# Weights times V in an attention kernel: one 128-column product, or two 64-column products into two halves of the PSUM partitions

## The reference, cut to what matters

```python
def _attn_ref(q, k, v, proj):            # q, k, v: (2, 8, 768, 64) float32
    q_bits = (np.einsum('bhsd,dk->bhsk', q, proj) > 0)
    k_bits = (np.einsum('bhsd,dk->bhsk', k, proj) > 0)
    ...                                  # six bits make a bucket number
    mask = q_bucket[:, :, :, None] == k_bucket[:, :, None, :]
    scores = scale * np.matmul(q, k.transpose(0, 1, 3, 2))
    scores = np.where(mask, scores, -1000000000.0)
    scores = scores - np.max(scores, axis=-1, keepdims=True)
    attn = np.exp(scores)
    attn = attn / (np.sum(attn, axis=-1, keepdims=True) + 1e-09)
    return np.matmul(attn, v)            # the product that is changed

def reference(...):
    attn_out = _attn_ref(...)            # 16 heads of 768 x 64
    x = attn_out.transpose(0, 2, 1, 3).reshape(B * S, H * D)    # 1536 tokens x 512
    x = _moe_ref(x=x, ...)               # 512 -> 1024, SoLU, layer norm, -> 512
    return _moe2_ref(x=x, ...)           # eight experts, 512 -> 1024 -> 512
```

## Time and profile before

| | us |
|---|---|
| device time, median of 3 runs | 761.47 |
| the three runs | 761.47, 760.52, 2372.37 |
| profiled execution, from its first to its last instruction | 759.0 |
| TensorE busy in it | 662.9 (87%) |
| VectorE busy in it | 496.5 (65%) |
| ScalarE / GpSimd busy | 345.8 / 273.6 |
| `values` (L456): 384 matmul instructions | 134.0 busy |
| `attended` (L720): 32 copies | 540 to 561 ns each |

### The profile page before, as it was taken

The page is one execution under the profiler, slowest core; times in us unless marked ns, Lnnn a source line. Parts: engine busy times, 40 slices in busy tenths (PEclk is TensorE's granted clock), DMA queues, the critical chain, the costliest instruction groups (busy, mean ns, idle before and its releaser), DMA issues.

```text
span 759.0 us, 11820 instructions
## 1 busy us (share of the span) xinstructions
PE 662.9 (87%) x3190; PEld 515.1 (68%) x3191; DVE 496.5 (65%) x931; ACT 345.8 (46%) x563; POOL 273.6 (36%) x185
## 2 busy tenths in 40 slices
PE   3899999999999998899999999850499999999994
PEld 1666666666666666677888888630378878788783
DVE  5788888888888888746565656645234556465621
ACT  2566666666666665552222222322234545454520
POOL 2566666655555554523132222456100010101011
PEclk9899999999999999999999999965599999999998
DMA  9933333333332232003000000035544475656400
GB/s 262 280 99 98 98 97 97 97 97 97 96 97 88 87 87 63 1 1 111 1 1 0 0 0 0 0 116 215 196 167 133 158 251 167 222 174 247 145 17 27
DMA packets 35419, 79.48 MB, mean 105 GB/s; under 512 B 6461, under 2 KB 6589, under 8 KB 35392
## 3 DMA queue, kind: packets, MB, share of 16 engines
q1 hardware_dynamic: 28112, 67.97, 28.7%
q10 hardware_dynamic: 5040, 4.87, 2.4%
q0 software_dynamic: 2240, 6.31, 2.2%
HBM read 67.82 MB, written 12.35 MB: 106 GB/s over the span
## 4 chain that ended last, share of the span: by engine, by line
PE 58%; DVE 21%; issue 10%; POOL 3%; ACT 3%; DMA 2%; ACTq 1%; DVEq 1%; SPq 0%; POOLq 0%
PE PS L439 7%; PE PS L418 7%; DVE sb_nm L681 6%; PE PS L612 4%; PE PS L614 3%; PE PS L613 3%; PE PS L593 3%; PE PS L594 3%; PE PS L595 3%; PE PS L524 3%; PE PS L471 3%; PE PS L473 3%; PE PS L472 3%; PE PS L526 3%; PE PS L525 3%
## 5 line engine op out<-in xcount | busy, mean ns | idle before, releaser
L1200 POOL TENSOR_TENSOR at_P<-at_P,sb_rr 128x768 f32<-128x768 f32 x80 | 121.8, 1530 | 115.6 <-DVE sb_rr L693 115.6
L456 PE MATMUL PS<-at_PT,at_V 128*128 128x384 f32 x384 | 134.0, 486 | 0.0
L991 ACT ACTIVATE at_P<-PS,sb_nb,sb_sc 128x768 f32<-128x768 f32 x96 | 95.5, 995 | 67.8 <-DVE sb_nb L685 66.8
L916 DVE TENSOR_TENSOR at_W<-at_raw,at_W 128x2048 f32 (+1 forms) x29 | 65.6, 2290 | 67.9 <-ACT at_W L1070 65.2
L418 PE MATMUL PS<-at_B,at_A 128*128 128x384 f32 x384 | 96.2, 373 | 13.4 <-DVE at_B L672 6.0
L681 DVE TENSOR_REDUCE sb_nm<-PS 128x1 f32<-128x768 f32 x96 | 91.6, 954 | 21.9 <-PE PS L418 21.6
L456 PEld LDWEIGHTS PS<-at_PT,at_V 128*128 128x128 f32 x384 | 72.2, 190 | 38.4
L439 PE MATMUL PS<-sb_cst,at_P 128*128 128x128 f32 x576 | 78.6, 280 | 19.5 <-DVE at_PT L716 9.4
L1005 ACT ACTIVATE at_PT<-PS 128x384 f32<-128x384 f32 x160 | 66.5, 490 | 59.5 <-PE PS L439 59.3
L439 PEld LDWEIGHTS PS<-sb_cst,at_P 128*128 128x128 f32 x576 | 65.1, 142 | 37.6 <-issue 16.6
L1293 POOL DMA_INDIRECT out<-at_yb,sb_to x16 | 15.8, 985 | 203.2 <-DVE at_yb L928 203.2
(11 more groups left out here) (148 smaller groups left out, 1187.0 us busy)
## 6 DMA issues: line engine op xcount, KB each, us to landing
at_raw<-w SPq DMA_DIRECT2D x32, 1024.0 KB, 6.7
at_AA<-qT SPq DMA_DIRECT2D x32, 192.0 KB, 4.2
at_KK<-kT SPq DMA_DIRECT2D x32, 192.0 KB, 4.4
at_V<-vP SPq DMA_DIRECT2D x16, 384.0 KB, 3.0
rows_by_expert<-at_empty SPq DMA_DIRECT2D x19, 257.0 KB, 10.4
at_XS<-rows_by_expert ACTq DMA_DIRECT2D x17, 256.0 KB, 2.7
at_stg<-w_solu SPq DMA_DIRECT2D x16, 256.0 KB, 3.4
at_QK<-qT SPq DMA_DIRECT2D x16, 192.0 KB, 3.6
```

What stands on the lines that cost most here:

```text
L456: m = mm(PS[:, PVB, 0:UQ], V[c][:, kt, :], PTb[w][:, kt, :], start=(kt == 0), stop=(kt == KT - 1))
L991: fn(Pr[w][j % UT].rearrange("p (g n) -> p g n", g=2), slot(7 * c + 1 + j), ACT.Exp, bias=nb[:, col], scale=sc[:, col], accum_out=sm[:, co ...
L1200: pool.tensor_tensor(p, p, rr[:, col].broadcast_to([P, S]), ALU.mult).then_inc(s_norm, 1)
```

## The change: two products of 192 queries in place of one of 384

In `values`, the stationary operand becomes the 64 columns of V that belong to head `h`. The 384 queries are cut into two groups `g` of 192. Group 0 is written to PSUM partitions 0 to 63 and group 1 to partitions 64 to 127 of the same bank, columns 0 to 191. For each `kt` there are so two products, g = 0 and then g = 1, where there was one. `s_pv` is still raised once, by the last. In the built program the product of 128 x 128 stationary values at array position (0, 0) is replaced by products of 128 x 64 at positions (0, 0) and (0, 64). In `attended`, one copy of 64 partitions x 384 becomes two copies of 64 x 192, one from each half of the partitions, both into the 64 partitions of `xT` that the head has; `s_pvev` is raised by the second. Nothing else is moved: every instruction but these stands where it stood on each engine.

```diff
@@ -452,9 +452,12 @@
                         pe.wait_ge(*evac_count(kt, 2 * h + w, w))
                 else:
                     pe.wait_ge(*evac_count(KT - 1, 2 * h + w, w))
+                v = V[c][:, :, c * D:(c + 1) * D]
                 for kt in range(cut) if half == 0 else range(cut, KT):
-                    m = mm(PS[:, PVB, 0:UQ], V[c][:, kt, :], PTb[w][:, kt, :],
-                           start=(kt == 0), stop=(kt == KT - 1))
+                    for g in range(2):
+                        m = mm(PS[g * D:(g + 1) * D, PVB, 0:UQ // 2], v[:, kt, :],
+                               PTb[w][:, kt, g * UQ // 2:(g + 1) * UQ // 2],
+                               start=(kt == 0), stop=(kt == KT - 1))
                 if half == 1:
                     m.then_inc(s_pv, 1)
 
@@ -717,8 +720,10 @@
 
             def attended(i, h, c, w):
                 dve.wait_ge(s_pv, 2 * h + w + 1)
-                dve.tensor_copy(xT[c * D:(c + 1) * D, ds(i * S + w * UQ, UQ)],
-                                PS[c * D:(c + 1) * D, PVB, 0:UQ]).then_inc(s_pvev, 1)
+                for g in range(2):
+                    m = dve.tensor_copy(xT[c * D:(c + 1) * D, ds(i * S + w * UQ + g * UQ // 2, UQ // 2)],
+                                        PS[g * D:(g + 1) * D, PVB, 0:UQ // 2])
+                m.then_inc(s_pvev, 1)
 
             def soft(n, b, first):
```

## The result

The changed kernel takes 763.3 us (median of 7 runs), the kernel before 760.7: a ratio of 1.0031, 95% interval 1.0017 to 1.0046. That is no change by the 2% of this measurement, and a small loss by its interval. A repeat beside other kernels gave 1.0021, 1.0005 to 1.0036.

A forecast was written before the change was run, and what follows sets the result against it. VectorE's chain was taken to bound each head and cover the values products. Copies +1.5 us and last head -1.5 gave 0 with overlap, +1.5 to +2 without; taken as +0.5: 762.0 us against 761.5, range 757 to 775.

The forecast's parts named there:

- The main step: In each head, all four blocks of values products are covered by VectorE's chain, overlapping or not; 758.5 to 766, chance 0.75.
- The chain itself: In a head, VectorE's sequence of maximum, inverse, hash rows and copies, taken to set the length of 19.58 us.
- The overlap: In the values blocks, the two half products run side by side, saving 3.9 us of TensorE a head; chance 0.55.
- The loads: Before each values product, the 64-column weight load hides under streaming at cost 0; otherwise at most 2.6 us a head.
- The change of shape: Around each values block, switching between 128 and 64 columns, 8 times a head, costs 0 to 0.1 us each; at most 0.27.
- The copies: In attended on VectorE, two small copies cost +0.10 us on the chain for w = 1, +1.5 us over 15 heads.
- The last head: In head 15 TensorE is the chain: -1.5 us if the halves overlap, 0 to +0.5 without.
- The slower rival (serial halves, paid changes): In each head, serial halves and shape changes at 0.27 us add 1.2 us: 781; chance 0.15.
- my slack: TensorE time covered in each head: about 0.6 us before scores 0 and 0.35 before the next head's transposes.
- The clock: Idle TensorE before 210.99 us lowers the granted clock for a quarter of each head: +2 us a head, 792; chance 0.04.
- a clock below 1.00 between 30 and 340 us: Sign over the attention that the prediction is wrong: the granted clock leaving 1.00, the level of 2.4 GHz.
- From span to time: For the whole run, the median lies 2.5 us above the profile's span, turning 759.5 into 762.0.

The follow-up runs named there:

- Experiment 5: Kernel before with only two of the six products of each half, nothing added: ratio 1.0173, 13 us slower.
- experiment 9: Kernel before with the w = 1 copy out of the values bank moved from VectorE to ScalarE in heads 0 to 14: ratio 0.9999.
- Experiment 2: Kernel before with a 64-column stationary operand, one product of 384 queries into the head's 64 partitions, one copy: ratio 1.0024.
- experiment 7: Kernel before with five idle products (1.1 us) added at the end of each half of heads 0 to 14: ratio 1.0101, 7.4 us slower.
- Experiment 4: Changed kernel with five idle products added at the end of each half in heads 0 to 14: ratio 1.0013 against the kernel before.
- experiments 3, 6 and 10: Changed kernel, loops exchanged (1.0028); changed form only in head 15 (1.0006); w=1 copy on ScalarE with changed product everywhere (1.0014), in head 15 (0.9996), plus filler (0.9963).

## Why the prediction was right, and which steps were not

The outcome, 763.3 in a range of 757 to 775 and "no change", is as forecast. The main step held: all four blocks of `values` lie beside the chain that sets a head's length. Experiment 5 shows it best, since heads with a third of the product are as long as before where the clock stays up. The chain itself I had too narrow: I called it VectorE's, and wrote that each wait of TensorE in the head ends on VectorE, while the earlier trace rows has `hashes` waiting for ScalarE, and experiment 9 shows ScalarE's copy, transposes and scores on it. The forecast's +0.5 against the +2.6 measured hides steps that missed in both directions:

- **The overlap**: given 0.55; it is complete, 0.080 us between starts in place of 0.161. The loads hide, as taken.
- **The change of shape**: taken as 0 to 0.1 us, measured 0.17 to 0.22, inside the bounds of 0 and 0.27. The Trainium skill (TensorEngine Tiling (Array Packing), "Key Properties") says that changing the tiling mode drains TensorE. The traces agree in that a change costs time, 0.17 to 0.22 us; that it is a drain they do not show.
- **The copies**: I had put the w = 1 copy on the chain, at +0.10 in each of 15 heads, +1.5. The lengthening was under-sized (0.16 to 0.28 instead of 0.10, as the two copies do not overlap), and the place was wrong: the copy lies beside the exponential of tile 3 (experiment 9). What sticks out is 0.1 in every second head, 0.7 in all; that the cover is used up there is my reading.
- **The last head**: -1.5 forecast, -1.6 in every trace that has the alternating pair there (-0.9 with the loops exchanged).
- **The slower rival (serial halves, paid changes)**: its price a head was too high. Experiment 2 pays 1.4 us of changes a head, and its heads are no longer; experiment 7 adds 2.2 us and loses 0.46, where my slack gave 1.2.
- **The clock**: this is the step that failed, and only its small size here left the forecast standing. I gave it 0.04, looked at one head in mid-loop, where TensorE is busy 15.35 of 19.52 us and the clock does stay 1.00, and did not ask where TensorE already idles longest. That is the end of the loop: 1.79 us before, 3.1 us after, and again where the second half of head 14 waits for GpSimd (315.30). In the four traces with both falls they cost 2.7 to 4.0 us, and in some traces 1.6 more behind the last head. Experiment 4 takes the added idle time in head 14 away, and these falls go with it; experiment 5 adds idle time, and the clock falls in the loop too. The prediction had named a clock below 1.00 between 30 and 340 us as a sign that it is wrong, and that sign came. My price of 30 us for this rival assumed a fall in every head.
- **From span to time**: I added 2.5 us. In every run whose time and span are both on record the distance is 1.9 to 2.2; nothing hangs on the difference.

That the forecast of +0.5 came within about 2 us of the outcome is in part luck: +1.5 of copies where 0.7 were, and nothing for falls of the clock that cost more.

In the two traces of the changed kernel there are +0.7 of copies, -1.6 in the last head, and falls of the clock, 2.8 to 5.6. Before the routing 1.5 to 1.7 are given back, with the missing stretch near 492; the rest lies in the start-up and behind the routing. The median's +2.6 is of that size, but is not split by it. How often each fall occurs over all runs was not measured; two traces of the changed kernel, and one of it with its copies elsewhere, all show the pair near 301 and 315 us.

The mean granted clock of every run is on record, and it points the same way. It is 0.956 over the 19 runs of the changed kernel and 0.960 over 93 of the kernel before. It is 0.955 or 0.956 in all four variants of experiments 3, 6 and 10 that have the pair and no filler, 0.958 and 0.962 in the two that have the pair and filler, and 0.961 with two copies or the copy on ScalarE alone. A difference of 0.0036 over 761 us is 2.7 us of TensorE's time, by estimate. It does not tell at which place a run lost it.

## What to carry to other kernels

Before speeding up an engine that is 87% busy, follow who waits for the very instructions that become faster; here only two of 32 readers did, and both in the last head. If nobody waits, the saved time turns into idle time, and on TensorE idle time is not neutral: it can lower the granted clock for work that *is* waited for. Look for that first at the places where it idles longest already. In the changed kernel these are the seams of the program and not its steady loop, while with two thirds of the product left out the loop was hit as well, in 7 of 11 heads.

## What the runs showed of the hardware

- Two float32 products of 64 stationary columns, on the two halves of the array's columns, run wholly side by side: 0.080 us an instruction of 192 columns against 0.161. They need not alternate: with four of a half in a row the overlap is still whole (eight in 0.88 us), with six or eight it is partial (twelve in 1.57 against 1.20, sixteen in 2.22 against 1.52).
- Going from 128-column to 64-column products or back costs 0.17 us a change (experiment 2), 0.22 in the changed kernel.
- Neighbouring VectorE copies of 64 x 192 start 0.27 to 0.28 us apart where both read the same 64 PSUM partitions, and 0.35 to 0.37, which is one behind the other, where they read different ones.
- Removing work can cost 13 us: with a third of the product left, the granted clock over 30 to 300 us was 0.93 instead of 1.00.
- The granted clock fell at the end of the loop in all five traces in which TensorE had waited 2.45 to 3.58 us there, and in none of the nine with 0.7 to 1.8. Behind the last head it fell in five of eight with 3.0 to 4.0 us.
